# Pair 0 of an attention and two-FFN kernel: first load in two halves, scores and maxima by head, gate copies on ScalarE

## The reference

```python
scores = scale * np.matmul(q, k.transpose(0, 1, 3, 2))      # causal mask, softmax over the keys
a /= a.sum(-1, keepdims=True) + 1e-09
local = np.matmul(a, v)
q_p = phi(q)                                                # phi(x) = where(x > 0, x, exp(x) - 1) + 1
mem_out = (q_p @ M_prev) / (q_p @ z_prev + 1e-06)
g = 1.0 / (1.0 + np.exp(-beta))                             # one gate for each head
attn = g * mem_out + (1 - g) * local
x = moe(tokens(attn))                                       # silu(x @ w_gate) * (x @ w_val) @ w_out
out = moe2(x)                                               # clipped-square unit of (x @ w_in), @ w_out
```

## Time and profile before

| | us |
|---|---|
| median of 3 runs (lowest, highest) | 977.68 (976.7, 978.08) |
| the profiled execution, its own time | 977.74 |
| its span in the trace | 975.9 |
| TensorE busy | 964.4 (99%) |
| VectorE / ScalarE / GpSimd busy | 694.1 / 459.5 / 335.8 |
| granted TensorE clock, all 40 slices | 9 of 10 or more |

### The profile page before, as it was taken

The page is one execution under the profiler, slowest core; times in us unless marked ns, Lnnn a source line. Parts: engine busy times, 40 slices in busy tenths (PEclk is TensorE's granted clock), DMA queues, the critical chain, the costliest instruction groups (busy, mean ns, idle before and its releaser), DMA issues.

```text
span 975.9 us, 19122 instructions
## 1 busy us (share of the span) xinstructions
PE 964.4 (99%) x6372; PEld 926.9 (95%) x6372; DVE 694.1 (71%) x1369; ACT 459.5 (47%) x940; POOL 335.8 (34%) x385
## 2 busy tenths in 40 slices
PE   8999999999999999999999999999999999999998
PEld 7878778999999999999999999999999999999998
DVE  6888999486667555557555568888887677867766
ACT  7899888554444232233222236545543333433331
POOL 5777775287781000100001157688410010000000
PEclk9999999999999999999999999999999999999999
DMA  7555542697768655555555544767785744538321
GB/s 248 168 170 164 154 158 99 244 325 295 280 238 313 237 209 219 220 220 213 203 194 198 211 150 149 250 236 268 287 267 211 268 187 170 221 136 301 141 104 65
DMA packets 46158, 204.74 MB, mean 210 GB/s; under 512 B 5488, under 2 KB 5872, under 8 KB 46064
## 3 DMA queue, kind: packets, MB, share of 16 engines
q1 hardware_dynamic: 45920, 203.52, 57.8%
q10 hardware_dynamic: 144, 0.00, 0.0%
HBM read 147.33 MB, written 56.17 MB: 209 GB/s over the span
## 4 chain that ended last, share of the span: by engine, by line
PE 89%; DVE 4%; issue 2%; POOL 2%; ACT 2%; DMA 1%; SPq 0%; DVEq 0%; ACTq 0%; POOLq 0%
PE ps L1485 26%; PE ps L1486 25%; PE ps L1487 25%; PE ps L1434 5%; PE ps L1405 4%; PE ps L1458 3%; DVE negs L1079 1%; ACT rown L821 1%; POOL wu_l L720 1%; PE ps L1381 0%; DMA rbc<-rsums 0%; PE ps L1415 0%; DVE norms L1064 0%; ACT wu_h L850 0%; DVE xt_l L1140 0%
## 5 line engine op out<-in xcount | busy, mean ns | idle before, releaser
L1485 PE MATMUL ps<-xt_h,wu_h 128*128 128x384 f32 x840 | 281.3, 335 | 0.4 <-DVE wu_l L1131 0.2
L1487 PE MATMUL ps<-xt_h,wu_l 128*128 128x384 f32 x840 | 280.7, 334 | 0.0
L1486 PE MATMUL ps<-xt_l,wu_h 128*128 128x384 f32 x840 | 280.7, 334 | 0.0
L1485 PE MATMUL ps<-hid_h,wd_h 128*128 128x384 f32 x672 | 225.2, 335 | 2.4 <-DVE xy L1258 1.5
L1487 PE MATMUL ps<-hid_h,wd_l 128*128 128x384 f32 x672 | 224.6, 334 | 0.0
L1486 PE MATMUL ps<-hid_l,wd_h 128*128 128x384 f32 x672 | 224.5, 334 | 0.0
L1258 DVE TENSOR_TENSOR xy<-xy,ps 128x384 f32<-128x384 f32 x288 | 158.4, 551 | 69.2 <-PE ps L1487 69.0
L935 ACT ACTIVATE hid_h<-hid_r 128x768 fp32r<-128x768 f32 x84 | 70.8, 843 | 205.3 <-DVE hid_r L1232 140.2
L1485 PEld LDWEIGHTS ps<-xt_h,wu_h 128*128 128x128 f32 x840 | 157.6, 188 | 2.5 <-issue 0.9
L1486 PEld LDWEIGHTS ps<-xt_l,wu_h 128*128 128x128 f32 x840 | 157.7, 188 | 0.0
L1487 PEld LDWEIGHTS ps<-xt_h,wu_l 128*128 128x128 f32 x840 | 157.7, 188 | 0.0
(11 more groups left out here) (87 smaller groups left out, 1291.9 us busy)
## 6 DMA issues: line engine op xcount, KB each, us to landing
wu_l<-kept_ul SPq DMA_DIRECT2D x40, 896.0 KB, 7.6
wu_h<-kept_uh SPq DMA_DIRECT2D x40, 896.0 KB, 5.5
kept_uh<-wu_h SPq DMA_DIRECT2D x20, 896.0 KB, 6.1
kept_ul<-wu_l SPq DMA_DIRECT2D x20, 896.0 KB, 7.4
wd_h<-kept_dh SPq DMA_DIRECT2D x28, 512.0 KB, 3.8
wd_l<-kept_dl SPq DMA_DIRECT2D x28, 512.0 KB, 5.2
wu_r<-w_up SPq DMA_DIRECT2D x20, 512.0 KB, 5.5
qk<-qk_in SPq DMA_DIRECT2D x15, 640.0 KB, 5.1
```

The lines of the kernel that those rows point to most:

```text
L1485: nc.tensor.matmul(dst, w_hi, v_hi, start=start, stop=False, skip_group_check=onto)
L1486: nc.tensor.matmul(dst, w_hi, v_lo, start=False, stop=False, skip_group_check=onto)
L1487: return nc.tensor.matmul(dst, w_lo, v_hi, start=False, stop=stop, skip_group_check=onto)
```

## The change

The first load is cut by heads: partitions 0 to 63 on SyncE's queue and 64 to 127 on ScalarE's. The rest of qk 0 moves to ScalarE's queue, ahead of beta. In pair 0 TensorE makes tile 4 of head 0, then that of head 1, and VectorE takes each maximum behind its own. In all pairs `scores_f` and the scores of tile 3 wait for the first maximum of tile 4 and no longer for the second. VectorE takes all maxima of pair 0 ahead of `norm_q(0)` and `mem_scale`, and `phi(0)` ahead of the gates. The three copies into `gt` go to ScalarE, ahead of `exp_tile(1)`. Products of zeros become 7 at the start, then 2 and 6 in round 0 and 6 between the first scores and the first turn of round 1. (Context and moved lines cut.)

```diff
@@ sync: loads
-            sp.dma_start(qk[:, 0, cut:], qk_in[0][:, cut:]).then_inc(ld_first, 16)
+            sp.dma_start(qk[0:D, 0, cut:], qk_in[0][0:D, cut:]).then_inc(ld_first[0], 16)
             load_nat(0)
-            sp.dma_start(qk[:, 0, 0:cut], qk_in[0][:, 0:cut]).then_inc(ld_qk[0], 16)
             load_nat(1)
@@ scalar
+            act.dma_start(qk[D:P, 0, cut:], qk_in[0][D:P, cut:]).then_inc(ld_first[1], 16)
+            act.dma_start(qk[:, 0, 0:cut], qk_in[0][:, 0:cut]).then_inc(ld_qk[0], 16)
             act.dma_start(betas[:, 0], beta.rearrange("(o h) -> o h", o=1).broadcast_to([P, 2 * HPB])).then_inc(ld_beta, 16)
             act.wait_ge(ld_beta, 16)
@@ scalar, p == 0
                     exp_q(1)
+                    act.wait_ge(gexp_1, 1)
+                    heads = gexp[:, 0].rearrange("p (k o h) -> p k o h", o=1, h=2)
+                    nc.scalar.activation(gt[:, :, 1:].rearrange("p k (i h) -> p k i h", h=2),
+                                         heads.broadcast_to([P, NPAIR, SLOTS, 2]), ACT.Copy).then_inc(gt_set, 1)
+                    for h in range(2):
+                        half = slice(D * h, D * h + D)
+                        nc.scalar.activation(gt[half, :, 0:1], heads[half, :, 0, h:h + 1], ACT.Copy).then_inc(gt_set, 1)
+                    exp_tile(1)
                     act.wait_ge(gone_set, 1)
...
-                    for k in range(1, SLOTS):
+                    for k in range(1 if p > 0 else 2, SLOTS):
                         exp_tile(j + k)
@@ vector, tile_max
-                at_least(dve, scored, j + 2 if i == 2 else j + 1)
+                if j > 0:
+                    at_least(dve, scored, j + 2 if i == 2 else j + 1)
                 for h in range(2):
+                    if j == 0:
+                        dve.wait_ge((scored_first, scored)[h], 1)
@@ vector, ahead of the loop
+            dve.wait_ge(maskf_set, 2)
+            tile_max(0)
+            phi(0)
             dve.wait_ge(gexp_e, 2)
             nc.vector.tensor_scalar(gexp[:], gexp[:], 1.0, None, ALU.add).then_inc(gexp_1, 1)
             dve.wait_ge(gexp_1, 1)
-            (the three copies into gt, tile_max(0))
+            nc.vector.reciprocal(gone[:], gexp[:, 1]).then_inc(gone_set, 1)
             nc.vector.memset(cf[0:D, :, 0], 1.0).then_inc(cf_set, 1)
-            nc.vector.reciprocal(gone[:], gexp[:, 1]).then_inc(gone_set, 1)
-            phi(0)
-            tile_max(1)
+            for k in range(1, SLOTS):
+                tile_max(k)
@@ vector, loop
-                    tile_max(j + 2)
+                    if p > 0:
+                        tile_max(j + 2)
                     mem_scale(j)
                     mem_scale(j + 1)
-                    tile_max(j + 3)
+                    if p > 0:
+                        tile_max(j + 3)
@@ tensor
-            idle_products(10)
+            idle_products(7)
...
-                    at_least(pe, maxed, 2 * SLOTS * p + 2)
+                    at_least(pe, maxed, 2 * SLOTS * p + (1 if i == 3 else 2))
...
+            def scores_first():
+
+                i, w = SLOTS, width(SLOTS)
+                for h in range(2):
+                    rows = slice(D * h, D * h + D)
+                    col = score_col(i, h)
+                    pe.wait_ge(ld_first[h], 16)
+                    for a0, a1 in ((0, 512), (512, w)):
+                        mm = nc.tensor.matmul(psf[:, col + a0:col + a1], qk[rows, 0, P + q0(i):P + q0(i) + P],
+                                              qk[rows, 0, P + S + a0:P + S + a1], start=True, stop=True)
+                    mm.then_inc((scored_first, scored)[h], 1)
...
-                at_least(pe, maxed, 2 * SLOTS * p + 2)
+                at_least(pe, maxed, 2 * SLOTS * p + 1)
@@ tensor, loop
-                if p < NPAIR:
+                if p == 0:
+                    scores_first()
+                    idle_products(2)
+                elif p < NPAIR:
                     scores(SLOTS * p)
+                if p == 1:
+                    idle_products(6)
                 (turns of p - 1)
-                if p == 0:
-                    idle_products(4)
...
-                    idle_products(8)
+                    idle_products(6)
```

More of the change, by code:

```diff
@@ L153, in attention_two_ffns @@
         r_in = [sem(f"r_in{s}") for s in range(2)]
-        ld_first = sem("ld_first")
+        ld_first = [sem(f"ld_first{h}") for h in range(2)]
+        scored_first = sem("scored_first")
         r_row = sem("r_row")
@@ L871, in x_high @@
                 nc.scalar.activation(xt_h[:, n], src[n] if n in src else raw_sum(sb, n), ACT.Copy).then_inc(x_hi, 1)
+            cut = P + q0(SLOTS)
+            act.dma_start(qk[D:P, 0, cut:], qk_in[0][D:P, cut:]).then_inc(ld_first[1], 16)
+            act.dma_start(qk[:, 0, 0:cut], qk_in[0][:, 0:cut]).then_inc(ld_qk[0], 16)
             act.dma_start(betas[:, 0], beta.rearrange("(o h) -> o h", o=1).broadcast_to([P, 2 * HPB])).then_inc(ld_beta, 16)
@@ L1389, in scores @@
                 w, s = width(i), p % 2
-                if j == 0:
-                    pe.wait_ge(ld_first, 16)
-                else:
+                if j > 0:
                     at_least(pe, ld_qk[s], 16 * (p // 2 + 1))
```

## The result

The changed kernel takes 980.06 us (12 runs, 978.85 to 981.85) against 977.34 of the kernel before: ratio 1.0026, 95% interval 1.0019 to 1.0033. It is slower by 2.7 us where I forecast 977.4, and outside my range of 975.8 to 978.9. The profiled execution took 979.55, with a span of 977.7. The chains of the kernel before and of the changed one reach the networks at

A forecast was written before the change was run, and what follows sets the result against it. TensorE's dense stretch was taken to bound the kernel, so a shifted first turn carries to the end. A first turn 0.6 us later and 0.9 gained in the rounds made -0.3 on 977.74: 977.4 us, range 975.8 to 978.9.

The forecast's parts named there:

- M = B + 6.0: Pair 0: VectorE's last maximum (M) comes 6.0 us after beta lands (B), gated by ScalarE's work; M at 13.4.
- B = 7.4: Opening loads: beta, behind two large transfers on ScalarE's queue, lands at 7.4 us; ends of the range 5.6 and 8.4.
- One packet for one: Opening loads: when both queues hold work they pass packets about one for one, 110 together in a us.
- The first rival: Opening loads: beta lands in time, at 5.6 to 6.8 us, and VectorE's own order decides; 976.3 us; chance 0.25.
- Zero products of round 1 cost 0.7: Round 1: the six zero products end 0.7 us later than the first turn needs, so they set its start.
- 0.9 from the relaxed wait: Rounds 1 to 8 and 15: waiting for tile 4's first maximum gains 0.10 us each, 0.9 together; ends 0 and 1.1.
- Clock: Rival: after TensorE's rest from about 11.3 to 13.5 us, part of round 1 runs at 1.2 GHz; 979 to 983; chance 0.03.
- The split load useless, beta last: Opening loads: the halves land at 5.5 us like the whole, beta at 10.4; 980.4 us; chance 0.05.
- the lost overlap: Tile 4 of pair 0: heads one behind the other cost about 0.6 us of TensorE, hidden under the start.

## Why the prediction was wrong

By medians against the kernel before the loss comes apart like this: beta first, 10 opening products: -1.7. Beta last, and 22 zeros to hold the clock (two edits): +1.1, so **beta costs 2.8**, 2.1 to 3.8 by the scatter, some 0.3 of it perhaps those zeros. Clock let go (6 instead of 22 zeros): +2.3, so **the clock costs 1.2** there, just at the edge of the noise; with 7 opening products the same pair gives 2.2, and the kernel before 1.6. Seven opening products: +2.7, **0.4**, inside the noise.

These prices do not add in every order. Seven opening products cost 1.8 with beta first (-1.7 to +0.2) and 0.4 with beta last, where ScalarE's wait hides them; so with 7 of them, beta last and the clock held is only 0.4 above beta first. What holds in any order is the whole: from the changed kernel, beta issued first gives back 2.6, the wait moved back 3.9, and the loads of before with 10 opening products 3.9.

- **M = B + 6.0**: right. 15.01 - 9.43 = 5.6, and 13.57 - 7.98 = 5.6 in the execution with an early beta, by way of ScalarE as described. That ScalarE's wait is the place is shown by the run with the wait moved back.
- **B = 7.4**: the step that failed. It came at 9.43, beyond my end of 8.4. Put into my own sum it gives +2.65 - 0.9, 979.5 instead of 977.4. Of the 2.0 us, 1.3 were there before beta's turn: I let the halves land by 3.5 to 4.2 and the second came at 5.2, and the rest of qk 0 was through at 6.6 and not at 5.3. I had taken 110 packets a us from the start and then 0.40 MB a us; but ScalarE's queue passed 3 packets before 3.0 us, and from 3.5 to 5.0 the two queues moved 0.25 MB a us. The other 0.7 is beta's own stretch, 2.8 against the 1.8 to 2.6 I gave it. That beta was handed over at 2.23, behind 0.58 and 0.86 us of issuing, did not set this, since its queue was busy until 6.6. Why the loads start so differently from one execution to the next (beta at 7.98 with the same order) stays open.
- **One packet for one** held for beta's stretch (73 and 60 a us beside 95 and 66), but not between the large loads: 6 packets on ScalarE's queue beside 80 from 4.0 to 5.0, then 134 beside 52. So the counts do not say whether beta's share of a DMA engine went in one turn, as the Trainium skill has it (DMA: Bandwidth & Descriptors, Queues, rings and completion order). The first rival is out by beta's landing alone: it needed a B of 5.6 to 6.8.
- **Zero products of round 1 cost 0.7**: wrong in its kind. With the clock held they cost 0.2 by the traces and nothing that the medians show, because without them TensorE waits for ScalarE's first copy. I had costed ScalarE only up to M, not what it does after.
- **0.9 from the relaxed wait**: right in kind, somewhat too small. 0.93 to 0.82 in a round by the rows, and 0.8 in rounds 1 to 8; 1.4 us by the start of the networks and 1.3 by the medians of the run with the clock held, beyond my end of 1.1. Where the rest of it comes from is not traced.
- **Clock**: right place, wrong chance. I gave 0.03 with the argument that today's rest of 1.4 does no harm. A rest of 2.0, which my own sum had at 2.2, was followed by the low clock, and in 8 of 11 executions of that kernel the mean was below 1. I had put it at nothing in the sum; it was the second largest term, 1.2 to 2.2 us.
- **The split load useless, beta last**: the rival I gave 0.05 (B = 10.4, 980.4) came nearest in time and in mechanism: the second half landed at 5.2, where the rival had 5.5 for both, though the first landed at 4.2. That it also meets 980.06 is luck: its B was 1.0 too late and it had no term for the clock. On two transfers to disjoint partition halves the Trainium skill (DMA: Bandwidth & Descriptors, Rules for kernel authors) says "Don't bother". The runs agree in effect: with 10 opening products the loads of before do as well, within the noise, as the split ones with beta first (1.1 and 1.7 under).

So the time went to ScalarE waiting for 4 KB behind 464 KB, and to TensorE at the lower clock after the rest this made. What the change was otherwise worth, 1.1 to 1.7 us by the medians, shows when beta's wait is mended (with beta first, only with 10 opening products); with the clock alone held the kernel stays 0.5 above the one before. The relaxed wait by itself, with its rest filled, gives 1.3 of it, so that of the split load, the order of heads and maxima and the copies on ScalarE no gain is shown.

## What to carry to other kernels

A load of a few bytes that an engine waits for ahead of its work goes first on its queue, or the wait goes behind the work that does not need it: its packets wait for all that its queue holds ahead of them, and then they took as many slots here as large ones. When an edit lets TensorE finish a stage earlier, measure the rest it leaves: here leaving it unfilled gave back about half of the edit's gain (0.7 of 1.3, by medians). And cost a late engine past the first consumer, up to its next hand-over.

## What the runs showed of the hardware

- Head by head did not give head 0 first: eight products, issued as the four of head 0 and then the four of head 1, took 1.37 us against 1.30 interleaved, and VectorE started its first maximum only 0.1 behind the end of all (in the changed kernel, with head 1's half late, 0.3 ahead of it). I had priced the lost overlap at 0.6. The Trainium skill (TensorE: Matmul & The Clock Gate, What overlaps and what doesn't) has matmuls start and end in program order; by that head 1 would follow head 0's second pass and the eight would take far longer than interleaved. The measurement decides: two of the products start within 0.03 us, at 5.71, and the next two at 6.3, so when both halves are there, the two row halves run side by side in either order.
- The granted clock fell after a rest of 2.0 us in the profiled execution of the relaxed wait alone, and the mean clock was below 1 in 8 of that kernel's 11 executions. It was 1.00 in all runs listed for the kernel before, whose rest was 1.4 in its profile.
- The same 352 KB load landed 4.8 to 5.7 us after its issue from one execution to another, and beta, behind the same loads, at 7.7 to 9.7 us. With the 0.9 us by which the networks differ, each is as large as many of the differences looked for here; how much of a kernel's spread each makes was not measured.
